# Moving the preparation of the logits' weights into the attention steps, and a chunk's key and query loads ahead of two weight pieces, in a fused retention and mixture-of-experts kernel

## The reference

```python
state = gamma * state + outer(k[:, :, t], v[:, :, t])
y[:, :, t] = scale * einsum('bhd,bhde->bhe', q[:, :, t], state)
```

```python
g = s * maximum(x @ w_in, 0) ** 2 + b
x2 = g @ w_out
```

## Time and profile before

| what | value |
|---|---|
| median of three runs | 938.25 us |
| the profiled execution | 937.93 us |
| its span, first to last instruction | 936.1 us |
| TensorE busy | 926.4 us, 99% |
| VectorE busy | 516.7 us, 55% |
| ScalarE busy | 295.6 us, 32% |
| GpSimd busy | 233.7 us, 25% |
| granted TensorE clock | 0.999 |
| up product, matmuls of L1054 | 28% of the chain that ended last |

### The profile page before, as it was taken

The page is one execution under the profiler, slowest core; times in us unless marked ns, Lnnn a source line. Parts: engine busy times, 40 slices in busy tenths (PEclk is TensorE's granted clock), DMA queues, the critical chain, the costliest instruction groups (busy, mean ns, idle before and its releaser), DMA issues.

```text
span 936.1 us, 18553 instructions
## 1 busy us (share of the span) xinstructions
PE 926.4 (99%) x7461; PEld 748.6 (80%) x7461; DVE 516.7 (55%) x1216; ACT 295.6 (32%) x553; POOL 233.7 (25%) x216
## 2 busy tenths in 40 slices
PE   8999999999999999999999999999999999999997
PEld 6777777778777777777777777778998998999996
DVE  6775666565665465477577676761534434424420
ACT  3453444344343452010101010101434534534421
POOL 5232322232221000001110101001443643643611
PEclk9999999999999999999999999999999999999999
DMA  9996766656655569666666757284635635635500
GB/s 336 316 315 229 245 223 246 236 219 240 241 216 200 189 231 335 238 204 229 212 222 204 242 192 234 90 273 144 209 111 182 197 120 179 203 123 170 180 34 34
DMA packets 81316, 192.92 MB, mean 206 GB/s; under 512 B 8880, under 2 KB 17584, under 8 KB 81232
## 3 DMA queue, kind: packets, MB, share of 16 engines
q1 hardware_dynamic: 77200, 178.98, 56.7%
q0 software_dynamic: 3840, 12.59, 4.2%
q10 hardware_dynamic: 192, 0.19, 0.1%
HBM read 128.54 MB, written 63.18 MB: 205 GB/s over the span
## 4 chain that ended last, share of the span: by engine, by line
PE 95%; DVE 2%; DMA 1%; issue 1%; ACT 0%; POOLq 0%; POOL 0%; DVEq 0%
PE bank L1054 28%; PE bank L1162 28%; PE bank L1203 14%; PE bank L1218 14%; PE bank L987 3%; PE bank L897 1%; PE bank L1183 1%; PE bank L921 1%; PE bank L856 1%; PE bank L1085 1%; PE bank L885 1%; DMA staging<-in_w_in 1%; PE bank L861 1%; PE bank L957 0%; PE bank L1011 0%
## 5 line engine op out<-in xcount | busy, mean ns | idle before, releaser
L1054 PE MATMUL bank<-x,wi_hi 128*128 128x512 f32 x768 | 240.8, 395 | 0.0
L1054 PEld LDWEIGHTS bank<-x,wi_hi 128*128 128x128 f32 x768 | 141.7, 188 | 45.4 <-issue 10.9
L687 POOL TENSOR_TENSOR w_lo<-w_raw,w_hi 128x512 fp32r<-128x512 f32 x72 | 93.1, 1302 | 292.7 <-ACT w_hi L802 292.4
L1054 PE MATMUL bank<-x,wi_lo 128*128 128x512 f32 x384 | 149.6, 390 | 0.0
L1162 PE MATMUL bank<-wo_b,g_back 128*128 128x512 f32 x552 | 137.8, 399 | 0.0
L1289 DVE SCALAR_TENSOR_TENSOR u_sb<-u_sb,cst 128x512 f32<-128x512 f32 x96 | 78.3, 815 | 99.1 <-ACT u_sb L732 99.1
L802 ACT ACTIVATE w_hi<-w_raw 128x512 fp32r<-128x512 f32 x128 | 76.2, 635 | 162.3 <-DMA w_raw<-in_w 161.9
L732 ACT ACTIVATE u_sb<-bank 128x512 f32<-128x512 f32 x96 | 57.5, 598 | 185.3 <-PE bank L1054 185.3
L1162 PEld LDWEIGHTS bank<-wo_b,g_back 128*128 128x128 f32 x552 | 99.5, 189 | 18.5 <-issue 0.8
L1588 DVE TENSOR_TENSOR w_lo<-w_raw,w_hi 128x512 fp32r<-128x512 f32 x56 | 61.1, 1091 | 67.6 <-ACT w_hi L802 67.3
L1583 DVE SCALAR_TENSOR_TENSOR e_lo<-bank,e_hi 128x384 fp32r<-128x384 f32 x64 | 35.4, 554 | 95.2 <-ACT e_hi L833 94.9
(11 more groups left out here) (205 smaller groups left out, 1189.7 us busy)
## 6 DMA issues: line engine op xcount, KB each, us to landing
g_rows<-g_sb SPq DMA_DIRECT2D x96, 512.0 KB, 3.0
g_back<-g_rows SPq DMA_DIRECT2D x80, 512.0 KB, 3.6
w_raw<-in_w SPq DMA_DIRECT2D x128, 256.0 KB, 3.8
x_rows<-x SPq DMA_DIRECT2D x25, 256.0 KB, 5.1
g_back<-g_rows SPq DMA_DIRECT2D x16, 384.0 KB, 4.7
kT<-in_k_turned SPq DMA_DIRECT2D x22, 256.0 KB, 3.7
qT<-in_q_turned SPq DMA_DIRECT2D x22, 256.0 KB, 3.8
vin<-in_v SPq DMA_DIRECT2D x22, 256.0 KB, 4.2
```

Of the source, the lines that this page charges most:

```text
L687: pool.tensor_tensor(low, w_raw[:, (p * E_PIECES + n) % RAW, :], high.bitcast(F32), ALU.subtract).then_inc(w1_lo_done, 1)
L1054: last = pe.matmul(up[i % 2][:, :], w[:, t, fs], x[:, half, t, :], start=(t == 0 and n_ == 0), stop=(t == DT - 1 and n_ == 2))
```

## The change

The partial products, which stood alone in steps 2, 6, 10 and 13, now stand in the attention steps 4, 8, 11 and 14. Each is turned one such step later (8, 11, 14 and step 2 of block 1). Quad 0 goes from step 4 to step 8. In block 0 the order within a step becomes turn, partial product, quad, insert; in later blocks the quad still follows the insert, and the last turn comes ahead of the insert of step 2 of block 1. ScalarE copies the partial product ahead of the step's relu, and VectorE copies the turned part at the start of its step. The bias product goes from step 1 to step 3 of block 1, and its sum on VectorE from the start of step 0 to the end of step 2. In every later block ScalarE's partial copy goes from step 3 to step 4. The waits follow. The loads of pieces 1 and 2 of `w_turned` go one step later. In SP's queue at the start, `kin` of chunk 3 and then keys and queries of chunk 4, with the wait for `inc_done`, stand ahead of weight pieces 2 and 3.

```diff
-FIRST_QUAD_AT = {4: 0, 11: 1, 14: 2}
+FIRST_QUAD_AT = {8: 0, 11: 1, 14: 2}
-W_OG_PART_AT = {2: 0, 6: 1, 10: 2, 13: 3}
-W_OG_AT = {3: 0, 8: 1, 11: 2, 14: 3}
-TURNED_AT = {2: 1, 5: 2, 9: 3}
-BIAS_AT, CAST_AT, DIGITS_AT = (1, 1), (1, 1), (1, 4)
+W_OG_PART_AT = {(0, 4): 0, (0, 8): 1, (0, 11): 2, (0, 14): 3}
+W_OG_AT = {(0, 8): 0, (0, 11): 1, (0, 14): 2, (1, 2): 3}
+TURNED_AT = {3: 1, 6: 2, 9: 3}
+BIAS_AT, CAST_AT, DIGITS_AT = (1, 3), (1, 1), (1, 4)
...
-                if n == 4:
-                    sp.wait_ge(inc_done, 1)
-                elif n == 5:
+                if n == 5:
...
-            for i in range(STAGE):
+            for i in range(STAGE // 2):
                 load_piece(i)
+            load("kin", 3)
+            sp.wait_ge(inc_done, 1)
+            for name in ("kT", "qT"):
+                load(name, 4)
+            for i in range(STAGE // 2, STAGE):
+                load_piece(i)
+            for name in ("vin", "kin"):
+                load(name, 4)
...
-            load("kin", 3)
-            load_chunk(4)
...
+                    if (blk, f) in W_OG_PART_AT:
+                        w_og_copy(W_OG_PART_AT[blk, f])
                     relu(i)
...
-                    if blk == 0 and f in W_OG_PART_AT:
-                        w_og_copy(W_OG_PART_AT[f])
-                    if blk and f == LAST_QUAD_AT + 1:
+                    if blk and f == LAST_QUAD_AT + 2:
                         partial_copy(blk - 1)
                     if (blk, f) == CAST_AT:
                         act.wait_ge(const_in, 16)
-                        act.wait_ge(w_og_done, QUADS)
+                        act.wait_ge(w_og_parted, QUADS)
...
-                if CPB < n <= 2 * CPB + 1:
-                    pe.wait_ge(w_og_ready, max(n - CPB - 1, 1))
-                    pe.wait_ge(w_og_copied, min(n - CPB, QUADS))
+                if CPB < n <= 2 * CPB:
+                    pe.wait_ge(w_og_copied, n - CPB)
+                if CPB + 1 < n <= 2 * CPB + 1:
+                    pe.wait_ge(w_og_ready, n - CPB - 1)
...
-                pe.wait_ge(state_added, adds(CPB + 1 + c if c else CPB) + 1)
+                pe.wait_ge(state_added, adds(CPB + 1 + c) + 1)
...
-                pe.wait_ge(state_added, adds(2 * CPB) + 1)
+                pe.wait_ge(state_added, adds(2 * CPB + 1) + 1)
...
+                    if (blk, f) in W_OG_AT:
+                        w_og_turn(W_OG_AT[blk, f])
+                    if (blk, f) in W_OG_PART_AT:
+                        w_og_parts(W_OG_PART_AT[blk, f])
+                    if blk == 0 and f in FIRST_QUAD_AT:
+                        quad(0, FIRST_QUAD_AT[f])
                     if f in ATT_AT[blk]:
                         if blk and f > LOGITS_AT:
                             pe.wait_ge(logit_copied, blk)
-                        if blk == 1 and f == min(ATT_AT[1]):
+                        if blk == 1 and ATT_AT[1][f] == 1:
                             pe.wait_ge(bias_ready, 1)
                         insert((blk + 1) * CPB + ATT_AT[blk][f])
-                    quads = QUAD_AT if blk else FIRST_QUAD_AT
-                    if f in quads:
-                        quad(blk, quads[f])
-                    if blk == 0 and f in W_OG_PART_AT:
-                        w_og_parts(W_OG_PART_AT[f])
-                    if blk == 0 and f in W_OG_AT:
-                        w_og_turn(W_OG_AT[f])
+                    if blk and f in QUAD_AT:
+                        quad(blk, QUAD_AT[f])
...
-                    if (blk, f) == (1, 0):
-                        bias_total()
+                    if (blk, f) in W_OG_AT:
+                        w_og_copy(W_OG_AT[blk, f])
...
-                    if blk == 0 and f == min(W_OG_AT):
-                        w_og_copy(0)
...
-                        if blk == 0 and f in W_OG_AT:
-                            w_og_copy(W_OG_AT[f])
+                        if (blk, f) == max(W_OG_AT):
+                            bias_total()
```

## The result

The changed kernel takes 943.94 us, the median of four runs (943.78 to 944.01); the kernel before took 938.25 us beside it (937.86 to 938.88). The ratio is 1.0061 [1.0048, 1.0073]: 5.7 us slower. The prediction was 937.55 us with a range of 936.2 to 938.9: wrong in sign and outside the range. The profiled execution took 943.78 us with a span of 941.9.

A forecast was written before the change was run, and what follows sets the result against it. The prediction took TensorE, busy for 99% of the span, to bound the kernel. Gains of 1.6 + 0.3 us less losses of 0.7 + 0.5 gave 938.25 - 0.7 = 937.55 us, range 936.2 to 938.9.

The forecast's parts named there:

- these seams: Waits and interruptions in TensorE's sequence where the diff acts; costs on other engines counted only if TensorE comes to wait.
- my rivals: Three other outcomes: the start gains 0.55 us (20%), the gain is given back (14%), the copy never keeps up (6%).
- the one on the other side: Rival, 6%: ScalarE copies late in steps 8, 11 and 14, each increment waits about 1 us, 940.3 us.
- Edit 1: Partial products moved into attention steps: 1.6 us gained on TensorE, plus 0.3 from the wait at step 2.
- edit 2: New order inside attention steps: increments wait for copies in step 4 and step 2 of block 1, 0.7 us lost.
- The wait at step 4: In block 0, TensorE's increment waits 0.55 us for ScalarE's copy of the same step's partial product.
- at step 2 of block 1 the increment: Increment(9) waits 0.15 us for VectorE's copy of the last turn.
- Edit 3: Start's loads reordered: chunk 4's scores stop waiting, but piece 3 delays x_copy(3) and the first up matmul; 0.5 us lost.
- Given back: Rival, 14%: the gain goes to a late chunk 8 (0.4 us) and step 4 waiting for piece 7 (0.3): 938.2 us.
- The sum: Whole kernel: gains 1.6 + 0.3, losses 0.7 + 0.5, a net gain of 0.7 us.

The follow-up runs named there:

- e3: The changed kernel with the start's loads in the old order and packet boundaries moved by directives at step 2 of block 0 and step 5 of block 1: 937.78 us.
- e1: The changed kernel, work untouched, packet boundaries moved by directives at step 2 of block 0 and step 5 of block 1: 937.89 us, ratio 0.9997.
- e2: e1 with ScalarE's x_copy(3) ahead of weight pieces 2 and 3: 936.85 us, ratio 0.9986.
- a4: The changed kernel with the loads of w_turned pieces 1 and 2 in the steps of before: 944.56 us, ratio 1.0069.
- c1: The changed kernel, work untouched, packet boundaries moved by directives at step 6 of block 0 and step 5 of block 1: 938.92 us, ratio 1.0008.
- d1: The changed kernel, work untouched, with the first boundary-moving directive at step 7 of block 0: 938.77 us, ratio 1.0005.
- a1: The changed kernel with the start's loads in the order of before: 943.42 us, ratio 1.0065.
- c2: The kernel before, work untouched, directive at step 6 of block 0 moving packet boundaries into step 8's small matmuls: 943.71 us, ratio 1.0055.
- e4: The kernel before with directives at the same steps as e1, moving its boundaries by 10 instructions only: 938.22 us, ratio 1.0002.
- a2: The kernel before with only the start's load order changed to that of the change: 938.57 us, ratio 1.0006.
- d2: d1 with ScalarE's x_copy(3) ahead of weight pieces 2 and 3: 937.87 us, ratio 0.9998.
- b1 to b4: Boundaries moved by a directive ahead of the main loop: changed kernel 943.7 us; kernel before 950.94; changed with old load order 944.69; changed with x_copy(3) first 943.45.
- a3: The changed kernel with 86 tiny products, results unused, ahead of the main loop: 945.2 us, ratio 1.0074.

## Why the prediction was wrong

- **The step that failed** is the sentence "What a change outside these seams costs other engines is hidden unless TensorE comes to wait", as I used it: I asked for waits on engines and on loads only, and costed a longer run of small matmuls at the sum of its parts. TensorE's own instructions are a load as well. The edit put 359 of them in a row into step 8 (325 before) and 342 into step 2 of block 1 (277 before), and it moved the packet boundaries to 93 and 83 instructions into them. Missing term: +2.98 + 1.91 for the gaps, +1.53 for the clock behind the first, 6.4 us in all. That the copies and products of these steps keep their prices (turn 0.37, partial product 0.90, quad 0.86 us) was right; that nothing else waits was not. None of my rivals had this mechanism; the one on the other side (940.3 us, the copy never keeps up) did not happen, and no increment in steps 8, 11 or 14 of the changed kernel waited.
- Could it have been seen? The kernel before has no such gap, so its trace gave no price. But the page had the 59 packets of 0.97 MB, and its lines of PE and PEld the instructions.
- **Edit 1 and edit 2**, forecast -1.6 - 0.3 + 0.7 = -1.2 us: right in the traces, not told from nothing by the medians. In e3 the time from the first up matmul (21.82) to the insert at step 6 of block 1 (106.54) is 84.72 us, before 107.56 - 21.67 = 85.89: -1.17. In e1 and e2 (first up at 22.70 and 22.00) it is 84.94 and 85.03, -0.95 and -0.86. The median of e3 gives -0.45, and its interval (-1.4 to +0.3 us) holds both -1.2 and 0; its profiled execution (937.08 us) was one of its fastest. The wait at step 4 was 0.42 for 0.55 forecast; at step 2 of block 1 the increment takes 0.69 instead of 0.47, about 0.2 for 0.15.
- **Edit 3**, forecast +0.5: the mechanism was right (piece 3 late, x_copy behind it, first up matmul at 22.2). The start came at 22.26 and 22.23, and at 21.99 to 22.70 in a4, c1, d1 and e1. With the old order of loads it came at 21.67 to 21.93 in five traces (before, a1, c2, e3, e4), so the two medians are 22.25 and 21.79, 0.46 apart; single traces spread as much. The medians of the times give +0.34 (a2) and +0.11 (e1 against e3), neither told from nothing. That ScalarE's order is what makes it a loss is shown by e2: with x_copy(3) first the wait is gone and it is 1.04 us below e1. d2 is 0.90 below d1, but d1 also stands still longer for its instructions (0.96 us against 0.43 and 0.03).
- **Given back** (chunk 8, piece 7) did not happen: no wait on a load or for a piece after 23 us.
- **The sum** -0.7 us: the change without its gaps (e1) measured -0.34 us, interval -1.1 to +0.6, and by the account of the first trace -0.53. It holds within what this measurement can tell, which is not enough to tell it from 0. The error lay in one unlisted resource, and my range had no room for it.

## What to carry to other kernels

Count TensorE's instructions wherever small matmuls are gathered: two for each, 256 to a packet. A run that spends 256 instructions in 2 to 4 us, with one boundary 40 or more instructions inside it and the next one before its end, can stop for 0.3 to 4 us and, behind the longer gaps (2.65 and 3.79 us), pay again through the clock. Its sign is a gap in the middle of a group that "issue" released, with a q8 packet whose record begins 2.2 to 2.8 us before TensorE goes on. Such a cost depends on everything that stands ahead in the program, so an edit can look bad (or good) for reasons that have nothing to do with it: before judging it, move the boundaries (among long matmuls, just behind a boundary) and time it again.

## What the runs showed of the hardware

- A jump in TensorE's program costs nothing within 256 instructions or well after a boundary (e4: 938.22 against 938.23 us), but 4.5 to 5.1 us of idle time where it left a run of small matmuls for the next 256 (b1 to b4). By the packets the jump has no price of its own: the packet of the next 256 is recorded at 23.1 to 24.3 us in these four traces and at 24.1 in the kernel before. That kernel needs it at 27.8 us; the jump asks for it at 21.3 to 22.2, and TensorE goes on 2.7 us behind the record.
- The gap is not constant: from 0.3 us (a4's second) to 3.8 (c2), and 4.1 in a3's start, where no jump was taken. I did not try what sets how late the packet's record begins. The core's DMA engines were busy for 0.64 to 1.07 of the time around the first gap, and whether instruction packets stand behind data there is open. The 2.2 to 2.8 us behind the record are not data's: at the second gap no data moved from 99.0 to 100.5 us (last two numbers: DMA share, GB/s), and TensorE still went on 2.5 us after the record.

```profile
99.50:100.00 0.50, 0.50 (x6) 0.00 (x0) 0.50 (x2) 0.00 (x0) 0.50 (x1) 1.00 0.00 0
```

- The same wait stands in the start. In 12 of the 18 traces, of kernels of both kinds, TensorE stops for 0.3 to 0.7 us at the second boundary; in the profiled executions of before and after it does not. It is a part of the spread of the starts above. In c1:

```profile
18.95 0.45 PE L946 MATMUL bank<-early_qT,state 64*64 64x128 f32 x7 [0.46 <-issue]
```

- That a packet is requested as TensorE's reading crosses the boundary before is inferred from the pairing of packets and boundaries. The Trainium skill (Advanced Engine Details and Errata, ISA Cache) states 128 KB for TensorE and, in the next lines, only two lines of 16 KB. The gaps fit the two lines; no run here shows room for more.
- In the changed kernel, a3's logits and c2, the boundary ahead of the gap stood 40 to 93 instructions into its run. Boundaries within the first 30 did no harm (28 in the changed kernel's step 14, 19 and 26 in e1), save in d1 (11 in, 0.96 us). There the packet is recorded 0.8 to 2.1 us behind the matmul at the boundary, and 2.6 us ahead of it in the kernel before (90.9 for 93.5); at the deep ones it comes 1.6 to 3.5 us behind. A packet recorded ahead of the matmul shows that TensorE reads its instructions ahead of its matmuls. That it is less far ahead deep inside such a run would explain the difference, but the two ranges overlap, and the reading itself is not in the trace.
